# Seven strip products for eight in the first layers of two token blocks, and the first block alone under attention

## What is computed

```python
scores = np.where(keep, scale * q @ k.T, -1e9)      # 2 batches, 8 heads, 768 tokens, window 128, 4 sinks
x = softmax(scores) @ v                             # reshaped to 1536 x 512
g = x @ w_gate; x = (g / (1 + np.exp(-g)) * (x @ w_val)) @ w_out      # B, d_ff 1536
h = x @ w_in2; out = (np.maximum(h, 0) + alpha * np.minimum(h, 0)) @ w_out2   # C, d_ff 2048
```

## Time and profile before

| | us |
|---|---|
| median of 3 runs | 666.01 (665.6 to 667.31) |
| the profiled execution | 665.63 |
| its span in the trace | 663.9 |

### The profile page before, as it was taken

How to read it: one execution, slowest core, us unless ns; L and a number is a source line. 1 busy time by engine, 2 the same in 40 slices (tenths; PEclk the granted TensorE clock), 3 DMA queues, 4 the chain that set the end, 5 groups by cost and what they waited for, 6 DMA issues and landing times.

```text
span 663.9 us, 8595 instructions
## 1 busy us (share of the span) xinstructions
PE 646.4 (97%) x3192; PEld 511.2 (77%) x3192; DVE 360.3 (54%) x630; ACT 179.7 (27%) x458; POOL 186.8 (28%) x240
## 2 busy tenths in 40 slices
PE   8889989899999999999999999999999999999998
PEld 5567766676667788888888888888888888888886
DVE  5945564555644333343333467565757566665655
ACT  5656455635561111111111323111111111110100
POOL 7857852111110247740040050131313131300000
PEclk9999999999999999999999999999999999999999
DMA  8333251011000013310010010010101010000013
GB/s 279 114 128 96 80 176 49 17 33 66 0 1 1 32 41 95 103 51 32 1 42 22 1 48 17 16 48 17 48 17 47 17 48 17 1 0 1 0 64 127
DMA packets 22473, 33.03 MB, mean 50 GB/s; under 512 B 2112, under 2 KB 8256, under 8 KB 22432
## 3 DMA queue, kind: packets, MB, share of 16 engines
q1 hardware_dynamic: 22288, 32.23, 15.2%
q10 hardware_dynamic: 144, 0.26, 0.1%
HBM read 29.34 MB, written 3.15 MB: 49 GB/s over the span
## 4 chain that ended last, share of the span: by engine, by line
PE 89%; DVE 4%; ACT 4%; issue 2%; DVEq 0%; ACTq 0%
PE ffn_ps L1330 28%; PE att_ps L1330 19%; PE ffn_ps L1361 18%; PE att_ps L1361 14%; PE att_ps L1294 2%; PE att_ps L1258 2%; PE att_ps L1275 1%; ACT scratch L1401 1%; ACT L1401 1%; DVE scratch L1494 1%; PE att_ps L1368 1%; DVE top L1478 1%; DVE att_ps L1467 1%; PE ffn_ps L1294 1%; ACT L1421 1%
## 5 line engine op out<-in xcount | busy, mean ns | idle before, releaser
L1427 ACT ACTIVATE h_hi<-h_sb 128x512 fp32r<-128x512 f32 x84 | 53.1, 632 | 300.9 <-DVE h_sb L1535 221.6
L1178 POOL CAST w_hi<-raw_weights 128x512 fp32r<-128x512 f32 (+1 forms) x74 | 47.0, 636 | 273.2 <-PE ffn_ps L1330 139.3
L1330 PE MATMUL ffn_ps<-x_hi,w_hi 128*128 128x512 f32 x280 | 111.0, 396 | 0.6 <-DVE x_lo L1515 0.6
L1330 PE MATMUL ffn_ps<-x_hi,w_lo 128*128 128x512 f32 x280 | 109.1, 390 | 0.0
L1330 PE MATMUL ffn_ps<-x_lo,w_hi 128*128 128x512 f32 x280 | 109.0, 389 | 0.0
L1540 DVE TENSOR_TENSOR h_lo<-h_sb,h_hi 128x512 fp32r<-128x512 f32 x84 | 68.2, 811 | 53.4 <-ACT h_hi L1427 53.3
L1179 POOL TENSOR_TENSOR w_lo<-raw_weights,w_hi 128x512 fp32r<-128x512 f32 (+1 forms) x74 | 90.2, 1219 | 5.9
L1330 PE MATMUL att_ps<-x_hi,w_hi 128*128 128x512 f32 x184 | 71.6, 389 | 0.0
L1330 PE MATMUL att_ps<-x_lo,w_hi 128*128 128x512 f32 x184 | 71.6, 389 | 0.0
L1330 PE MATMUL att_ps<-x_hi,w_lo 128*128 128x512 f32 x184 | 71.6, 389 | 0.0
L1330 PEld LDWEIGHTS ffn_ps<-x_hi,w_lo 128*128 128x128 f32 x280 | 52.6, 188 | 11.3
(11 more groups left out here) (137 smaller groups left out, 1078.5 us busy)
## 6 DMA issues: line engine op xcount, KB each, us to landing
raw_weights<-pieces SPq DMA_DIRECT2D x74, 256.0 KB, 2.6
k_sb<-kt SPq DMA_DIRECT2D x12, 264.0 KB, 4.2
v_sb<-vt SPq DMA_DIRECT2D x12, 256.0 KB, 3.2
out<-scratch SPq DMA_DIRECT2D x12, 256.0 KB, 2.0
q_sb<-qt SPq DMA_DIRECT2D x11, 256.0 KB, 4.8
scratch<-vs SPq DMA_DIRECT2D x1, 384.0 KB, 4.9
q_sb<-qt ACTq DMA_DIRECT2D x1, 256.0 KB, 2.5
alpha<-alpha_t SPq DMA_DIRECT2D x1, 8.0 KB, 6.2
```

The costliest lines, as they stand in the source:

```text
L1178: chain(pool.tensor_copy(hi, raw[:, j % n_raw, at]))
L1330: last = pe.matmul(ps, w_parts[a][:, kk * P:(kk + 1) * P], x_parts[b][:, kk, t * TB:(t + 1) * TB], start=kk == 0 and (a, b) == (0, 0), sto ...
L1427: act.activation(h_hi[:, s % n_h, :], h_sb[:, s % 2, :], ACT.Copy).then_inc(hhi_done, 1)
```

## The change

Block 0 takes all of B during attention. Blocks 1 and 2 are then treated as a pair. For a pair of hidden tiles and the pair of blocks, a front product is a 2x2 block product (two tiles of features, two halves of the input width, two blocks of tokens), and Strassen's algorithm in the form with 15 additions makes it with seven products in place of eight. Each is a `strip`: one chunk of six matmuls. A set is seven strips, for one of gate, value (B) or front (C); there are 20 sets. Sums of token halves (T1 to T4) are made once per layer by `pair_sum` on DVE, `round_sum` on ACT and `rest_of_sum` on DVE. Sums of weight halves (S1 to S4) are made by POOL for every set (`sum_pieces`): behind the splits of two pieces stand four sums, each an addition, a rounding and a rest of half width. The seven results are combined by a copy on ACT (`keep`) and five additions on DVE (`mix`). C's activation is now two relu on ACT (L1988, L1990) and one operation on DVE (L2187), all from SBUF for three of the four tiles of a set; B's product on DVE is L2182, the rest of a hidden tile L2193, the addition to the accumulator L2202 (the first one, a copy, L2218). Front groups that block 0 and the pair use at different times are loaded and split twice: 118 pieces in place of 74. All backs use the same two banks of PSUM.

The diff, cut to what the prediction speaks of:

```diff
+    STRIPS = (("A11", "B11", 0), ("S2", "T2", 1), ("A12", "B21", 0), ("S3", "T3", 1), ("S1", "T1", 2),
+              ("A22", "T4", 1), ("S4", "B22", 2))
+    N_STRIPS, N_MIXES = len(STRIPS), 5
...
+    n_alone = 5
...
+            g, part, i = key
+            m = (g, part)
+            h11, h12, h21, h22 = ((g, f, t) for f in range(F) for t in pair)
+            mixes = [("mix", (m, n)) for n in range(N_MIXES)]
+            if i == 0:
+                emit(chunk, [("keep", m)])
+            elif i == 1:
+                emit(chunk, [mixes[0]])
+            elif g[0] == "B" and part == 0:
+                emit(chunk, {2: [("silu", h11)], 3: [mixes[1]], 4: [mixes[2], ("silu", h22)],
+                             5: [mixes[3], ("silu", h21)], 6: [mixes[4], ("silu", h12)]}[i])
+            elif g[0] == "B":
+                emit(chunk, {2: [("hidden", h11)], 3: [mixes[1]], 4: [mixes[2], ("hidden", h22)],
+                             5: [mixes[3], ("rest", h11), ("hidden", h21)],
+                             6: [mixes[4], ("rest", h22), ("hidden", h12)]}[i],
+                     *([[("rest", h21), ("rest", h12)]] if i == 6 else []))
+            else:
+                emit(chunk, {2: [("relu", h11)], 3: [mixes[1], ("hidden", h11)],
+                             4: [mixes[2], ("relu", h22), ("rest", h11)],
+                             5: [mixes[3], ("hidden", h22), ("relu", h21)],
+                             6: [mixes[4], ("relu", h12), ("hidden", h21), ("rest", h22)]}[i],
+                     *([[("hidden", h12), ("rest", h21)], [("rest", h12)]] if i == 6 else []))
...
+    for n in range(at_join):
+        plan += emit_slot(slot(next_w, early, n_units))
+        next_w += 1
+    for chunk in backs(last_b):
+        emit_chunk(chunk)
+        plan.append(("x2", (single, chunk[1][2])))
+    for n in range(at_turn):
...
+    fill = (fronts(groups_c[1], 0) + fronts(groups_c[1], 1) + backs(groups_c[0])
+            + fronts(groups_c[2], 0) + fronts(groups_c[2], 1) + backs(groups_c[1]))
+    for n, chunk in enumerate(fill):
+        emit_chunk(chunk)
+        if n % 2 == 0 and steps:
+            plan += steps.pop(0)
+    for n, g in enumerate(pair_b):
         if n == 0:
...
+        if n + 1 < len(pair_b):
+            for chunk in strips(pair_b[n + 1], 0) + pair_backs(g) + strips(pair_b[n + 1], 1):
+                emit_chunk(chunk)
...
+    steps = sums_of("C")
+    for chunk in fronts(groups_c[3], 0) + fronts(groups_c[3], 1):
+        emit_chunk(chunk)
+    for t in pair:
+        for d in range(4):
+            emit_chunk(("back", (pair_b[-1], t, d)))
+            if t == pair[0] or d >= half_k:
+                plan.append(("x2", (t, d)))
...
+                plan.append(("tsum", ("C", 0, d)))
+    steps = steps[1:]
+    for n, chunk in enumerate(backs(groups_c[3]) + fronts(groups_c[4], 0) + fronts(groups_c[4], 1)):
+        emit_chunk(chunk)
+        if n in (0, 2, 4, 6, 7):
+            plan += steps.pop(0)
+    waiting = backs(groups_c[4])
+    for g in groups_c:
+        for chunk in strips(g, 0):
+            emit_chunk(chunk)
+            if steps:
+                plan += steps.pop(0)
+        for chunk in waiting:
+            emit_chunk(chunk)
+        waiting = pair_backs(g)
+        if g[1] >= n_alone:
+            for chunk in fronts(g, 0) + fronts(g, 1) + waiting:
+                emit_chunk(chunk)
+            waiting = backs(g)
+    for chunk in waiting:
+        emit_chunk(chunk)
...
-        def back_ps(k, d):
-            return bank(ffn_ps if k < dense or d < 2 else att_ps, 2 + d % 2)
...
+        def strip_ps(m, role):
+            return (bank(att_ps, 3), bank(ffn_ps, 0), bank(ffn_ps, 1))[role] if kind_of(m) == "V" else bank(att_ps, role)
+        def back_ps(key):
+            return bank(ffn_ps, 2 + back_no[key] % 2)
...
+                if i == 0:
+                    s = part_sum[:, 0, :]
+                    chain(pool.tensor_tensor(s, a21, a22, ALU.add))
+                elif i == 1:
+                    s = part_sum[:, 1, :]
+                    chain(pool.tensor_tensor(s, part_sum[:, 0, :], a11, ALU.subtract))
+                elif i == 2:
+                    s = part_sum[:, 0, :]
+                    chain(pool.tensor_tensor(s, a11, a21, ALU.subtract))
+                else:
+                    s = part_sum[:, 0, :]
+                    chain(pool.tensor_tensor(s, a12, part_sum[:, 1, :], ALU.subtract))
+                hi, lo = (w[:, (left, right)[i % 2]] for w in cell(name))
+                chain(pool.tensor_copy(hi, s))
+                pool.tensor_tensor(lo, s, hi.bitcast(F32), ALU.subtract).then_inc(split_done, 1)
...
+                first = i in (0, 1, 4)
+                if first:
+                    wait_for_bank(m, role)
+                elif i == 2:
+                    pe.wait_ge(kept_done, keep_no[m])
+                else:
+                    pe.wait_ge(mix_done, mix_no[m, {3: 0, 5: 1, 6: 2}[i]])
+                ps = strip_ps(m, role)
+                w_parts = cell(operand_cell(g, part, a_name))
+                b_parts = operands[b_name]
+                for kk in range(half_k):
+                    for a, b in PASSES:
+                        last = pe.matmul(ps, w_parts[a][:, block_cols(at * half_k + kk)], b_parts[b][:, kk, :],
+                                         start=first and kk == 0 and (a, b) == (0, 0),
+                                         stop=kk == half_k - 1 and (a, b) == (1, 0), skip_group_check=True)
+                last.then_inc(front_done, 1)
...
+                    for f in range(F):
+                        pe.wait_ge(split_done, job_no["piece", piece_key(g, f, part, t)])
+                        pe.wait_ge(hlo_done, rest_no[g, f, t])
+                if back_no[g, t, d] > 2:
+                    pe.wait_ge(evac_done, back_no[g, t, d] - 2)
+                ps = back_ps((g, t, d))
...
+                    if (f, t) == (0, pair[0]):
+                        act.wait_ge(front_done, strip_no[g, 0, 2])
+                        wait_for_value_tile(("keep", (g, 0)), TILE[f, t])
+                    else:
+                        act.wait_ge(mix_done, mix_no[(g, 0), {(1, 2): 2, (1, 1): 3, (0, 2): 4}[f, t]])
+                act.activation(gate_of(h), c11_of(h, 0), ACT.Relu).then_inc(relu_done, 1)
+                act.wait_ge(relu_done, 2 * relu_no[h] - 1)
+                act.activation(hidden_sb(h), c11_of(h, 0), ACT.Relu, scale=-1.0).then_inc(relu_done, 1)
...
+                if n == 0:
+                    dve.wait_ge(kept_done, keep_no[m])
+                    wait_for_tile(m, U_TILE)
+                    ins = dve.tensor_tensor(u, beta, p1, ALU.add)
+                elif n == 1:
+                    wait_for_tile(m, V_TILE)
+                    ins = dve.tensor_tensor(v, beta, p1, ALU.add)
+                elif n == 2:
+                    dve.wait_ge(mix_done, mix_no[m, 1])
+                    ins = dve.tensor_tensor(v, gamma, v, ALU.add)
+                elif n == 3:
+                    dve.wait_ge(mix_done, mix_no[m, 1])
+                    ins = dve.tensor_tensor(p1, beta, p1, ALU.add)
...
+                    dve.wait_ge(mix_done, mix_no[m, 0])
+                    ins = dve.tensor_tensor(u, gamma, u, ALU.add)
+                ins.then_inc(mix_done, 1)
...
+                g, f, t = h
+                if g[0] == "B":
+                    dve.wait_ge(silu_done, silu_no[h])
+                    if t == single:
+                        dve.wait_ge(front_done, front_no[g, f, 1])
+                        ahead = single_ahead(("hidden", h), f)
+                        if ahead:
+                            dve.wait_ge(hlo_done, rest_no[ahead])
+                    elif (f, t) == (0, pair[0]):
+                        dve.wait_ge(front_done, strip_no[g, 1, 2])
+                        wait_for_tile((g, 1), TILE[f, t])
+                    else:
+                        dve.wait_ge(mix_done, mix_no[(g, 1), {(1, 2): 2, (1, 1): 3, (0, 2): 4}[f, t]])
+                    dve.tensor_tensor(hidden_sb(h), c11_of(h, 1), gate_of(h), ALU.mult).then_inc(prod_done, 1)
+                else:
+                    dve.wait_ge(alpha_done, 1)
+                    dve.wait_ge(relu_done, 2 * relu_no[h])
+                    col = g[1] * F + f
+                    dve.scalar_tensor_tensor(hidden_sb(h), hidden_sb(h), minus_alpha[:, col:col + 1], gate_of(h),
+                                             ALU.mult, ALU.add).then_inc(prod_done, 1)
```

More of the change, by code:

```diff
@@ new lines, in build_windowed @@
+    made = {}
+    at = -1
+    for what, key in plan:
+        if what in ("front", "back", "strip"):
+            at += 1
+        elif what == "hidden":
+            made["h", key] = at
+    busy_until = {n: -1 for n in range(n_cells + n_h)}
+    cell_of, cell_ahead = {}, {}
+    start = {}
+    due = len(chunks)
+    for name in reversed(wanted):
+        due = min(due, used[name][0])
+        start[name] = due
```

(2 more changed lines are left out.)

968 lines of the change are left out of this document (690 added, 278 removed).

## The result

759.79 us, the median of four runs (756.59 to 763.72), against 665.84 before: ratio 1.141, 95% interval 1.134 to 1.147. The change makes the kernel 14% slower, and the time lies outside the range. The profiled execution has a span of 760.3 us.

What follows compares the result with a forecast made beforehand. The prediction took TensorE as the bound, waiting for nothing after attention. From the profiled 665.6 us, less 27.2 for removed matmuls, plus 61.5 of waits and 4 in attention, it forecast 704 us, range 674 to 722.

Steps and rivals of the forecast that it cites:

- What bounds the kernel now: After attention TensorE waits for nothing, so removing 120 matmuls gains 27.2 us if it goes on without waiting.
- The chains: Mostly after attention, strips and backs wait on accumulations, copies and sums late in DVE's and ACT's queues: 61.5 us.
- The bare chain of C: In each C set, queued DVE and ACT work delays third and fourth backs: 1.93 us, without delays from POOL.
- a gate set: In B, behind a value set, the third strip waits for `keep`: 1.18 us without POOL's delays, 3.0 with, five times.
- The fill: In the 16 chunks after attention, the third and fourth back of two groups wait: 6 us.
- The port: DVE and POOL lock each other out of SBUF; an exposed DVE operation waits 0.42 us in C, 0.49 in B.
- the forecast's rival without it: The same waits after attention without POOL holding DVE off: 36.4 us of waits, 679 us in all; chance 0.20.
- share of time: DVE's mean delay of 0.12 us at POOL 22% busy, scaled to 76% in C (0.42 us) and 90% in B.
- The clock: Longer waits bring TensorE to 1.2 GHz in five sets, 9.5 us more per 42 matmuls: 752 us; chance 0.03.
- if the granted clock leaves 1.00: Sign in the profile after: the prediction fails if TensorE's granted clock drops below full speed, 1.00.
- Attention: Same chunks and slots in another order; two slots without chunks between them and block 0's roundings cost +4 us, 0 to 9.
- the prediction's sign was 208 to 217: Sign in the profile after: attention, in the sense of the 76th chunk, ends at 208 to 217 us.

Runs made afterwards that it cites:

- filled waits: The changed kernel plus matmuls nobody reads: ten before the third strip of five gate sets, six before the third back after layer C's strips; 746.8 us.

## Why the prediction was wrong, point by point

**What bounds the kernel now: right.** TensorE had no wait to give, and 120 matmuls fewer are 27.2 us less.

**The chains: right.** Each place of the sum waited, for what the text named and about as long: 67.2 us against 61.5. The bare chain of C was 1.93 us a set in the hand working and is 1.99 in the trace, that of a gate set 1.18 and 1.05. The fill was mis-sized, 10.2 us against 6: its first wait alone, on block 0's first accumulation in C, was 6.4. There VectorE and ACT held each other up in turn: ACT's relu of the second tile (243.82 us) stood behind its rounding of two sums (242.69), these sums on VectorE behind the first tile's product (241.30), and the second tile's product (245.13) and the accumulation behind that relu.

**The port: right in mechanism and size.** A set of C was forecast at 3.4 us and lost 3.3, a gate set 3.0 and 3.1. Taken out, waits fall to 33.4 us; the forecast's rival without it had 36.4. Only the way there, by share of time, was rough. The Trainium skill, "SBUF — State Buffer", section "SBUF: two separate sides", tells of an exclusive lock between VectorE and GpSimd; the runs agree: an accumulation from PSUM kept its mean of 0.685 to 0.689 us in all of them, 40 of the changed kernel that started beside a GpSimd operation lost nothing, and an operation with two inputs from SBUF lost what GpSimd's had still to run, less 0.14 us.

**The clock: this step failed.** I gave it 0.03 as a rival, at five places of 42 slow matmuls each, and left it out of the range. The rows of before held no long wait from which to read it, and I took that as evidence that it would not come; with waits of 3 us forecast at a dozen places, it was a question of its own. It came at thirteen places after attention, but with 5 to 13 slow matmuls each, 1.2 to 2.7 us, not 9.5: 24.9 us in all. In this execution waits of 1.7 us and less that stood alone had none behind them, those of 2.8 and more always, and of the five between 2.0 and 2.5 two. By the prediction's own sign, "if the granted clock leaves 1.00", it failed. The Trainium skill, "TensorE: Matmul & The Clock Gate", section "Why this matters for your kernels", warns that an idle TensorE loses its clock; the filled waits show it on this kernel, with 21 us of slow matmuls less for the same waits.

**Attention: this step failed too.** "I take +4, from 0 to 9" stands against 24.4. Three terms are missing in it. The rest of x, one place earlier in VectorE's queue in the first 16 units (5.8 us by the first front, 3.7 of them waits): in the order of before it stood behind the next slot, which I had not compared. At the join I counted 1.4 us twice from a unit's scores to its exponentials, but not the product and rest of the last hidden tile ahead of the slot's mask, nor ACT's two table loads of 1.28 us between silu and exponential: 4.4 us of stall. At the turn a slot's mask (219.46 us) stands behind accumulations and rests of block 0's new x that wait for ACT's roundings in turn: 3.3 us. And the slow matmuls, which are the clock again: 5.4 us in chunks in three places, some 3 in attention's smaller matmuls and the other 2 ahead of the first front, some 10 of the 24.4 us. Attention ended at 232.1 us where the prediction's sign was 208 to 217.

The sum closes: 704, and 24.9 for the clock, 20.4 for attention, 5.7 for waits and 8.4 for other steps, less the 1.3 that the kernel before had of the last two, are 762.1 us, and the profiled execution took 762.06. The median is 2.3 lower. Of the other steps I forecast none; why a strip takes 1.38 us and not 1.36 is open.
